# ScalarE's softmax steps at fixed items of a round, and a token list with 64-byte entries

## The reference

```python
# attention: q, k, v are (4, 8, 576, 64)
scores = scale * np.matmul(q, k.transpose(0, 1, 3, 2))
kth = np.partition(scores, -top_k, axis=-1)[..., -top_k:-top_k + 1]
scores = np.where(scores >= kth, scores, -1000000000.0)
scores = scores - np.max(scores, axis=-1, keepdims=True)
attn = np.exp(scores)
attn = attn / (np.sum(attn, axis=-1, keepdims=True) + 1e-09)
x = np.matmul(attn, v)                      # -> (2304, 512)
# maxout
h = np.maximum(np.maximum(x @ w1, x @ w2), x @ w3)
x = h @ w_out
# experts
logits = x @ w_gate + modality_bias[modality_id]
e_idx = np.argmax(logits, axis=1)
for e in range(E):
    h = np.maximum(x[mask] @ w1[e], 0.0)
    out[mask] = gate_w[mask, None] * (h @ w2[e])
```

## Time and profile before

| | us |
|---|---|
| median of three runs | 996.27 |
| the three runs | 994.59, 996.27, 997.49 |
| the profiled execution | 994.58 |
| its span, first to last instruction | 993.0 |

### The profile page before, as it was taken

One profiled execution on the slowest core, in us unless ns is written; L12 is line 12 of the kernel. 1 busy time (PEld: TensorE's weight loads), 2 busy tenths in 40 slices (PEclk: granted clock), 3 DMA queues, 4 the chain that ended last, 5 costly groups with the idle time before them and its releaser, 6 DMA issues.

```text
span 993.0 us, 17993 instructions
## 1 busy us (share of the span) xinstructions
PE 920.3 (93%) x5324; PEld 680.3 (69%) x5325; DVE 716.7 (72%) x2191; ACT 570.0 (57%) x1226; POOL 656.5 (66%) x622
## 2 busy tenths in 40 slices
PE   4598789999999999999999999999989999989995
PEld 1254658577676667576676676675865998988894
DVE  4999999999999999999999999994404521331210
ACT  2577778777777677777776776775315122332211
POOL 7899988987887887888788877974253321221121
PEclk9999979999999999999999999999999999999998
DMA  5811112111112121212221121111054161143110
GB/s 199 245 57 56 54 39 64 54 56 57 52 56 67 56 57 51 63 49 58 61 56 56 41 67 58 39 36 36 12 95 139 27 219 52 42 136 118 42 53 32
DMA packets 60695, 69.69 MB, mean 70 GB/s; under 512 B 8064, under 2 KB 41984, under 8 KB 60608
## 3 DMA queue, kind: packets, MB, share of 16 engines
q1 hardware_dynamic: 56688, 58.40, 20.0%
q0 software_dynamic: 3920, 10.27, 3.3%
HBM read 59.05 MB, written 9.60 MB: 69 GB/s over the span
## 4 chain that ended last, share of the span: by engine, by line
PE 68%; issue 11%; ACT 10%; DVE 5%; POOL 2%; ACTq 0%; DVEq 0%; POOLq 0%
PE m_ps L1328 13%; PE m_ps L1405 10%; PE m_ps L1349 9%; PE s_ps L1388 7%; PE s_ps L1273 6%; PE m_ps L1342 6%; PE t_ps L1285 6%; PE o_ps L1301 4%; DVE top L1088 3%; ACT probs L884 2%; PE o_ps L1388 2%; ACT below L876 2%; PE m_ps L1356 1%; ACT probsT L913 1%; DVE upper L1090 1%
## 5 line engine op out<-in xcount | busy, mean ns | idle before, releaser
L746 POOL TENSOR_TENSOR scores<-scores,below 128x576 f32<-128x576 f32 x144 | 199.5, 1413 | 91.9 <-ACT below L876 91.8
L1328 PE MATMUL m_ps<-xT,w_sb 128*128 128x192 f32 x1152 | 200.8, 330 | 0.2 <-POOL w_sb L768 0.2
L1328 PEld LDWEIGHTS m_ps<-xT,w_sb 128*128 128x128 f32 x1152 | 188.4, 192 | 1.1 <-issue 1.1
L1088 DVE MAX8 top<-upper 128x8 f32<-128x288 f32 x384 | 159.5, 448 | 14.3 <-POOL lower L701 14.3
L1285 PEld LDWEIGHTS t_ps<-ident,probs 128*128 128x128 f32 x720 | 81.2, 143 | 64.8 <-issue 61.2
L1090 DVE MATCH_REPLACE8 upper<-top,upper 128x288 f32<-128x288 f32 x288 | 125.4, 444 | 0.0
L1285 PE MATMUL t_ps<-ident,probs 128*128 128x128 f32 x720 | 109.2, 283 | 14.0 <-ACT probsT L913 13.6
L884 ACT ACTIVATE probs<-scores,shift 128x576 f32<-128x576 f32 x144 | 112.3, 788 | 15.7 <-issue 12.5
L1273 PE MATMUL s_ps<-k_sb,q_sb 64*64 64x288 f32 (+1 forms) x576 | 101.6, 460 | 15.3 <-POOL ident L709 6.1
L754 POOL TENSOR_SCALAR probs<-probs,inverse 128x576 f32<-128x576 f32 x144 | 105.3, 751 | 13.6 <-DVE inverse L1071 13.6
L913 ACT COPY probsT<-t_ps 128x640 f32<-128x640 f32 x192 | 103.1, 563 | 18.2 <-PE t_ps L1285 16.5
(11 more groups left out here) (202 smaller groups left out, 1706.2 us busy)
## 6 DMA issues: line engine op xcount, KB each, us to landing
k_sb<-keys_t SPq DMA_DIRECT2D x48, 288.0 KB, 3.0
v_sb<-values SPq DMA_DIRECT2D x48, 256.0 KB, 2.7
raw<-e_w SPq DMA_DIRECT2D x12, 1024.0 KB, 5.1
q_sb<-queries_t SPq DMA_DIRECT2D x48, 96.0 KB, 1.9
maxout_rows<-x_rows SPq DMA_DIRECT2D x18, 256.0 KB, 2.0
w_sb<-w SPq DMA_DIRECT2D x2, 1536.0 KB, 10.5
v_sb<-values SPq DMA_DIRECT2D x48, 32.0 KB, 2.7
stage<-w_t SPq DMA_DIRECT2D x1, 1536.0 KB, 8.2
```

The costliest lines, as they stand in the source:

```text
L746: nc.gpsimd.tensor_tensor(scores[:, r % RING, i, :], scores[:, r % RING, i, :], below[:, i, :], ALU.subtract).then_inc(masked_ready, 1)
L1088: nc.vector.max(best, src).then_inc(topk_step, 1)
L1328: ins = nc.tensor.matmul(dst[:, a * BLK:(a + 1) * BLK], w_sb[:, w, c, (first + a) * P:(first + a + 1) * P], xT[:, m % 2, c, b % SPAN * BLK ...
```

## The change

ACT no longer uses shares. Each item gets a number (`places_in_round`), each step too, and a step goes ahead of the first item with a larger number. In every pass r the order is now: Q0, u1, V, Q1, H0, u2, e0, e1, the first M group, e2, the rest of the first half, H1, Q2, H2, the rectify steps, the other M groups but the last, then the scalars and u0 of round **r** (not r-1: they were the first steps of pass r+1), and the last M group. If the second half has no M group, scalars and u0 end the pass. A Y group isn't copied, so a step "behind" it stands right behind the item before.

List entries become 16 float32 (64 bytes), the last 14 zero. The list in HBM grows from 144 KB to 1152 KB; the fill repeats a tile 8 times for each partition. POOL zeroes 15 of the 16 columns of `empty` and `places` with two memsets. `fetch` still reads 8 bytes of an entry.

```diff
-WORK = {"Q": 1.2, "H": 0.8, "V": 1.8, "A": 2.7, "X": 5.3, "Y": 3.5, "T": 0.5, "L": 0.9, "W": 5.3}
-SOFTMAX_AT = (0.0, 0.0, 0.08, 0.16, 0.3, 0.42, 0.54)
-RECTIFY_AT = 0.7
+UNDER_1, UNDER_2, EXP, LAST_EXP, RECTIFY, NEXT = 0, 3, 3, 4, 7, 9
+ENTRY = 16
+FILLS = 8
+def places_in_round(r):
+    items = round_items(r)
+    first = {"Q0": 0, "V": 1, "Q1": 2, "H0": 3, "H1": 6, "Q2": 7, "H2": 7}
+    after_h1, seen, at = 0, 0, []
+    for item in items:
+        if item[0] == "M":
+            seen += 1
+            at.append(9 if after_h1 else 4 if seen == 1 else 5)
+            continue
+        name = item[0] if item[0] == "V" else f"{item[0]}{item[1]}"
+        after_h1 = after_h1 or name == "Q2" or name == "H1"
+        at.append(first[name])
+    if items and items[-1][0] == "M":
+        at[-1] = 10
+    return list(zip(items, at))
...
-        self.places = sb("places", [P, T, 2])
+        self.places = sb("places", [P, T, ENTRY])
-        self.empty = sb("empty", [P, E * CAP // P, 2])
+        self.empty = sb("empty", [P, E * CAP // P // FILLS, ENTRY])
...
-            sp.dma_start(list_dram.rearrange("(p n) c -> p n c", p=P), shared.empty[:, :, :]).then_inc(routing_in, 16)
+            sp.dma_start(list_dram.rearrange("(p a n) c -> p a (n c)", p=P, a=FILLS),
+                         shared.empty[:, :, :].rearrange("p n c -> p (n c)").unsqueeze(1)
+                         .to_broadcast([P, FILLS, E * CAP // P // FILLS * ENTRY])).then_inc(routing_in, 16)
...
-            nc.gpsimd.memset(shared.empty[:, :, 1:2], 0.0).then_inc(empty_ready, 1)
+            nc.gpsimd.memset(shared.empty[:, :, 1:ENTRY], 0.0).then_inc(empty_ready, 1)
+            nc.gpsimd.memset(shared.places[:, :, 1:ENTRY], 0.0)
...
-                nc.gpsimd.dma_start(info[:, :, :], list_dram[bass.ds(row, CH), :].rearrange("(n p) c -> p n c", p=P))\
+                nc.gpsimd.dma_start(info[:, :, :], list_dram[bass.ds(row, CH), 0:2].rearrange("(n p) c -> p n c", p=P))\
...
             def one_round(r):
-                steps, at = [], []
+                steps = []
                 if in_range(r - 1):
-                    steps, at = softmax_steps(r - 1), list(SOFTMAX_AT)
+                    _, _, under_1, under_2, exp_0, exp_1, exp_2 = softmax_steps(r - 1)
+                    steps += [(UNDER_1, under_1), (UNDER_2, under_2), (EXP, exp_0), (EXP, exp_1), (LAST_EXP, exp_2)]
...
+                if in_range(r):
+                    steps += [(NEXT, step) for step in softmax_steps(r)[:2]]
+                ran = 0
+                for item, at in places_in_round(r):
+                    while ran < len(steps) and steps[ran][0] < at:
+                        steps[ran][1]()
                         ran += 1
```

More of the change, by code:

```diff
@@ L178 @@
 TURN_AT = {("X", 1): (0,), ("T", 1): (1,), ("T", 2): (2,)}
-def work_done(items):
-    work = np.cumsum([WORK[item[2][0] if item[0] == "M" else item[0]] for item in items])
-    return [w / work[-1] for w in work]
+def places_in_round(r):
[13 more added lines that the diff above has]
+    return list(zip(items, at))
 class Shared:
@@ L959, in one_round @@
             def one_round(r):
-                steps, at = [], []
+                steps = []
                 if in_range(r - 1):
-                    steps, at = softmax_steps(r - 1), list(SOFTMAX_AT)
+                    _, _, under_1, under_2, exp_0, exp_1, exp_2 = softmax_steps(r - 1)
+                    steps += [(UNDER_1, under_1), (UNDER_2, under_2), (EXP, exp_0), (EXP, exp_1), (LAST_EXP, exp_2)]
                 for m, u in finished_units(r - 1) if r <= LOAD_AT else LAST_UNITS if r == RECTIFY_LAST else []:
-                    at.append(RECTIFY_AT if in_range(r - 1) else 0.0)
-                    steps.append(lambda m=m, u=u: rectify(m, u))
+                    steps.append((RECTIFY if in_range(r - 1) else -1, lambda m=m, u=u: rectify(m, u)))
                 if r == RECTIFY_LAST:
                     for n in range(PIECES):
-                        at.append(0.0)
-                        steps.append(lambda n=n: high_piece(0, n))
-                items, ran = round_items(r), 0
-                for item, done in zip(items, work_done(items)):
-                    while ran < len(steps) and at[ran] < done:
-                        steps[ran]()
+                        steps.append((-1, lambda n=n: high_piece(0, n)))
+                if in_range(r):
[4 more added lines that the diff above has]
+                        steps[ran][1]()
                         ran += 1
@@ L986, in one_round @@
                                 x_high_part(0, n)
-                for step in steps[ran:]:
+                for _, step in steps[ran:]:
                     step()
@@ L1460, in build @@
     x2_dram = nc.dram_tensor("maxout_rows", (TOKENS, D), F32).ap()
-    list_dram = nc.dram_tensor("dispatch_list", (E * CAP, 2), F32).ap()
+    list_dram = nc.dram_tensor("dispatch_list", (E * CAP, ENTRY), F32).ap()
     with ExitStack() as ctx:
```

## The result

The changed kernel took 998.8 us (median of 10 runs, 996.55 to 1001.99) against 995.39 us for the kernel before (10 runs), a ratio of 1.0035 with a 95% interval of 1.0024 to 1.0047. Forecast were 1000.3 us, or 4.0 us more than before; measured were 3.4 us more. The profiled execution took 998.04 us with a span of 996.4, so 3.4 us more than the one before by span as well. The total was right, and in part by luck: the terms for the [X | A] passes and for pass 12 came as forecast (1.4 and 0.4), the moved wait was priced 1 us too high and the start nearly 1 us too low, and a fall of the clock (+1.8) and a shorter wait behind attention (-2.2), which stood in no term, nearly cancelled.

What follows compares the result with a forecast made beforehand. DVE bounds the kernel up to about 150 us, PE from 200 to 650 us. Terms 1.2 + 1.4 + 0.4 + 1.1 = +4.1 us, 4.0 kept, on 996.3 give 1000.3 us; range 992 to 1004.5.

Steps and rivals of the forecast that it cites:

- [X | A] passes: Passes 15, 23, 31, 39: e2 replaces the shorter rectify step before H1's copy, H2 starts 0.34 us later; +1.4 us.
- The wait moves from Q1 to H2: Thirteen T,A passes: Q1 starts 0.61 us earlier, H2 0.09 us later with about 1 us wait; +1.2 us.
- Pass 12: At pass 12 the last M group's copy queues behind the threshold wait, delaying Q0's copy and PE; +0.4 us.
- The start: Start of kernel: last exponential of round 1 now behind W's copy, so DVE waits longer; +1.1 us, upper end 1.9.
- Masks and passes with Y: POOL's third mask comes 1 to 2 us later, at no cost; passes with Y first get no H2 wait.
- POOL drags: Rival: later third mask delays POOL's queue and the first divided tile for H0, adding 4 us: 1004.3; chance 0.15.
- The list: Larger memsets, list writes and reads beside PE's work cost nothing, except possibly at PE's wait at 738.64 us.
- the wait at 738: PE's wait of 3.58 us at 738.64, where POOL sends the 15 list writes; left unchanged in the sum.
- my own list of signs: Signs in the profile after; the prediction is wrong if H2's waits stay, Q1's stay, or the 738 us wait changes.
- The rival took the wait for one of the list's writes: Rival: larger entries end the 3.58 us wait at 738.64; gain at most 3.7 us before the gather; 996.7; chance 0.18.

Runs made afterwards that it cites:

- order_only: The changed kernel with 8-byte entries and the small fill, so ACT's new order alone; 998.2 us, ratio 1.0028 to the kernel before.
- u2_ahead: The changed kernel with the third mask step moved out of the stretch between Q1's and H1's copies to an earlier place; 982.4 us, ratio 0.9876.
- u2_again: u2_ahead run once more, unchanged; 992.0 us, ratio 0.9959 to the kernel before.
- list_again: list_only run once more, unchanged; 995.5 us, ratio 1.0001 to the kernel before.
- list_only: The kernel before with the 64-byte list and its fill alone, ACT's order the old one; 988.9 us, ratio 0.9936.
- e2_ahead: The changed kernel with the last exponential ahead of the copy of the first M group instead of behind it; 1005.4 us, ratio 1.0104.
- e2_filled2: e2_ahead with two repeated matmuls on PE ahead of H2 in each T,A pass; 1001.2 us, ratio 1.0045 to the kernel before.

## Why the prediction was right, point by point

- **The wait moves from Q1 to H2 (+1.2).** The move is right in place and size: 7.11 us from Q1 to H2, wait 0.95, in twelve of the thirteen passes (1.08 in pass 24). Pass 11 has a wait of H2 too, 0.90 us, which was not forecast. The net price is not 0.09 but about 0.01 us a pass. A T,A pass grew from 13.06 to 13.73 us, and the pass ahead of it, at whose end Q1's wait had stood, shrank by 0.63 to 0.73. I had taken the recorded idle time (0.61) as the gain, not the passes' lengths. The term was sized 1 us too large: 1.2 forecast, about 0.1 measured.
- **[X | A] passes (+1.4).** Right. Without the vanished wait of 0.66 us before Q1 such a pass would have fallen from 14.74 to 14.08; it took 14.45, 0.37 us for each of four passes.
- **Pass 12 (+0.4).** Right: Q1 begins 2.38 us later than before, of which 2.0 us come from the threshold. Only the wait by the profile is 0.66, not 0.85: V ended later too.
- **The start (+1.1, up to 1.9).** DVE waited 3.54 us for the last exponential, not 2, and the threshold of round 2 ended at 57.34 us instead of 55.33: +2.0. The named order of events is there (exponential behind W's copy, 54.13). But W began at 46.30 and not at 46.0, since H0 waited 1.57 us for the division, and took 7.31 us instead of 6.74. How far this is the change's doing the runs make doubtful: order_only ended that threshold at 55.42 us, and the same kernel ended it at 54.64 in u2_ahead and 57.84 in u2_again, with W at 5.77 and 7.47 us. The fault was to treat one execution as exact to a microsecond there. Two numbers of this step: 46.0 + 6.74 is 52.7 and not 52.6, and the 5 us in its estimate for the fill is not the 6.9 of its row and was given no source; the fill landed after 11.6 us, against 8.2 with the small fill in order_only, so that the 3.3 us of the estimate came out.
- **Masks and passes with Y (0).** Right: 14.83 or 14.84 us in those with Y in the first half, with no wait over 0.3 us for H2. The rival "POOL drags" did not happen; DVE's waits for sums rose from 21.5 to 24.0 us without any price.
- **The list (0) and the wait at 738 (left).** The list's 0 was right with the stall of ACT (list_again) and wrong by 6.6 us without it (list_only). In after's profile the stall was there, but shorter: PE waited 1.44 instead of 3.58 us, which by my own list of signs is a miss, and 2.2 us came back behind attention. The rival took the wait for one of the list's writes. That was wrong: order_only, with 8 bytes, had no such wait, and list_again, with 64, had it. But its bound was the right one: the gathered rows, due soon after, are what the entries' width can bring forward.
- **What was in no term:** the clock. One fall of 1.8 us in the profiled execution. The clocks of after's ten runs lie at 0.986 to 0.989, most of before's in the runs below at 0.986 to 0.990, so other runs may have such falls too; how much of the median they are is not shown.

The steady terms were forecast at 3.0 us (1.2 + 1.4 + 0.4) and were about 1.8 (1.4 + 0.4). To that came the start (2.0 in this profile, 1.1 forecast), the fall (1.8) and the shorter stall (-2.2): 3.4 us. The order of the steps and the waits that it makes were understood; that the total fits to 0.6 us is luck.

## What to carry to other kernels

A queue worked in order is a budget between two hand-overs: when a step is moved out of one gap, reckon the next gap with it in, and look for the step that can leave both (here the third mask step, 0.66 us in each T,A pass, which turned a loss of 2.0 us from pass 13 to 44 into a gain of 6.2). Waits of PE of about 1 us can be dearer than they look, because the clock can fall behind them: here 0.6 us of waiting, moved to another place, cost 1.8 us there in one pass. Before a gain of a few microseconds is put down to a change, run the same kernel again on another chip, and compare stretches that repeat (here passes 13 to 44, alike to 0.03 us for equal kernels) besides medians. Two late things can hide each other, so that taking away one of them shows nothing.

## What the runs showed of the hardware

- TensorE's granted clock fell to 1.2 GHz behind waits of 1.08 us (after, pass 24) and of 1.26 to 1.56 us (e2_ahead, 4 of 12 passes; in the others it stayed up behind 1.26 and 1.27 us). The wait stood between a group of 1.19 us and two of 0.74 and 0.96 us. With 0.89 us of extra matmuls in the wait (e2_filled2) it stayed up in all 12.
- The same kernel had medians of 982.4 and 992.0 us on two chips (and another kernel 988.9 and 995.5) while the kernel before took 995.5 and 996.9 (995.5 and 995.6). In the profiles some 8 us of the first difference lie in a stall of ScalarE behind attention and the low clock behind it, and 3.5 us ahead of pass 13.
- Beside scattered writes of 8 bytes 4 KB packets of another transfer took up to 4.7 us, and POOL stood 8.9 to 11.1 us before it could fetch from the list (three profiles); with 32 or 64 bytes no such packet took 2.5 us, and POOL stood 5.5 to 6.9 us (eleven profiles).
